# One load per group for chunk 0's queries and keys, chunk 1's groups on every second step, a third early expert

## The reference, cut to what matters

```python
# attention: 4 batches, 8 heads, 576 positions, head size 64, causal window of 64
scores = where((rel >= 0) & (rel < 64), q @ k.T / 8, -1e9)
x = softmax(scores) @ v                      # -> 2304 tokens x 512
# dense layer
h = x @ w_in                                 # 512 -> 2048
x = (h * tanh(softplus(h))) @ w_out          # 2048 -> 512
# routed layer, 8 experts of 512 -> 1024 -> 512
go  = x @ w_skip > 0                         # only these tokens are computed
e   = argmax(x @ w_gate); gate = softmax(x @ w_gate)[e]
out = x;  out[go] = x + gate * (relu(x @ w1[e]) @ w2[e])
```

## Time and profile before

| what | us |
|---|---|
| median of three runs (747.63 to 750.29) | 749.41 |
| the profiled execution | 753.54 |
| its span, first to last instruction | 752.0 |
| TensorE busy (92% of the span) | 693.8 |
| VectorE busy | 485.8 |
| ScalarE busy | 362.9 |
| GpSimd busy | 272.0 |

### The profile page before, as it was taken

One profiled execution on the slowest core, in us unless ns is written; L12 is line 12 of the kernel. 1 busy time (PEld: TensorE's weight loads), 2 busy tenths in 40 slices (PEclk: granted clock), 3 DMA queues, 4 the chain that ended last, 5 costly groups with the idle time before them and its releaser, 6 DMA issues.

```text
span 752.0 us, 13811 instructions
## 1 busy us (share of the span) xinstructions
PE 693.8 (92%) x4974; PEld 615.3 (82%) x4974; DVE 485.8 (65%) x920; ACT 362.9 (48%) x791; POOL 272.0 (36%) x238
## 2 busy tenths in 40 slices
PE   4867799999999999999999999997999889999993
PEld 3756679888888988988988988986888779999893
DVE  3453785686686686686687687678587635445360
ACT  4545445545555455455455555553454035353430
POOL 4415334344344434434335335334353232121221
PEclk9977999999999999999999999998999989999997
DMA  7624103116216415114215114101638789999940
GB/s 234 205 78 161 43 28 99 36 36 101 62 36 124 95 36 93 47 61 92 64 44 92 52 56 93 36 1 35 236 93 267 225 301 372 350 339 354 349 144 1
DMA packets 63410, 97.16 MB, mean 129 GB/s; under 512 B 23080, under 2 KB 28200, under 8 KB 63344
## 3 DMA queue, kind: packets, MB, share of 16 engines
q1 hardware_dynamic: 60176, 91.80, 41.2%
q0 software_dynamic: 3168, 4.51, 1.8%
HBM read 84.97 MB, written 13.73 MB: 131 GB/s over the span
## 4 chain that ended last, share of the span: by engine, by line
PE 73%; DVE 11%; DMA 5%; issue 4%; ACT 3%; POOL 1%; SPq 1%; POOLq 0%; DVEq 0%; ACTq 0%
PE Y L585 22%; PE H L566 14%; PE H L667 10%; PE OB L685 8%; PE PTB L566 6%; PE SB_ L531 4%; DMA tokens_of_experts<-tok_i,slot 3%; PE OB L550 2%; PE MB L613 2%; PE SB_ L539 1%; DVE n_sb L1008 1%; DVE u_sb L1019 1%; DVE u_sb L1015 1%; DVE g_sb L1024 1%; DVE u_sb L1004 1%
## 5 line engine op out<-in xcount | busy, mean ns | idle before, releaser
L1334 POOL TENSOR_TENSOR q_sb<-n_sb,r_sb 128x512 f32<-128x512 f32 x72 | 93.2, 1295 | 300.8 <-DVE u_sb L1019 223.3
L585 PE MATMUL Y<-wout_hi,g_hi 128*128 128x512 f32 x288 | 122.8, 427 | 16.1 <-ACT g_hi L803 16.0
L585 PE MATMUL Y<-wout_lo,g_hi 128*128 128x512 f32 x288 | 118.3, 411 | 0.0
L566 PE MATMUL H<-x_hi,win_hi 128*128 128x256 f32 x384 | 111.6, 291 | 0.0
L566 PE MATMUL H<-x_lo,win_hi 128*128 128x256 f32 x384 | 108.4, 282 | 0.0
L566 PE MATMUL H<-x_hi,win_lo 128*128 128x256 f32 x384 | 108.3, 282 | 0.0
L1340 POOL TENSOR_TENSOR g_lo<-g_sb,g_hi 128x512 fp32r<-128x512 f32 x72 | 95.4, 1325 | 0.8
L667 PEld LDWEIGHTS H<-xT,w 128*128 128x128 f32 x768 | 90.5, 197 | 1.9 <-issue 1.0
L667 PE MATMUL H<-xT,w 128*128 128x128 f32 x768 | 91.0, 281 | 0.8 <-ACT xT L828 0.8
L1004 DVE TENSOR_SCALAR u_sb<-e_sb 128x512 f32<-128x512 f32 x72 | 36.3, 504 | 84.3 <-ACT e_sb L788 83.8
L803 ACT CAST g_hi<-g_sb 128x512 fp32r<-128x512 f32 x72 | 44.6, 619 | 84.4 <-DVE g_sb L1024 76.4
(11 more groups left out here) (186 smaller groups left out, 1393.4 us busy)
## 6 DMA issues: line engine op xcount, KB each, us to landing
w<-moe_w SPq DMA_DIRECT2D x24, 2048.0 KB, 10.1
kT<-k_T SPq DMA_DIRECT2D x32, 256.0 KB, 3.0
vw<-v_w SPq DMA_DIRECT2D x32, 256.0 KB, 3.1
...
```

The lines of the kernel that those rows point to most:

```text
L566: last = nc.tensor.matmul(HM3[J % 3][:, f, :], wt[:, j, d, f * P:(f + 1) * P], xt[:, c % 2, d, :], start=(n == 0), stop=(n == 3 * DB - 1))
L585: last = nc.tensor.matmul(Y[t][:, :], gt[:, J % 2, lo:lo + P], wt[:, 2 * j + f, :], start=(j == 0 and f == 0 and wt is wout_hi and gt is g ...
L1334: nc.gpsimd.tensor_tensor(q_sb[:, :], n_sb[:, J % 2, :], r_sb[:, J % 2, :], ALU.mult).then_inc(q_ok, 1)
```

## The change

It has four parts.

1. **First loads.** Chunk 0's queries and keys lie side by side in one input (`qk0_T`), and come in one DMA for each group (`qk0`) in place of two; v is loaded from ScalarE's queue. SP issues 4 DMAs ahead of the first weight slices in place of 12, the slices come in another order, and GpSimd rounds four slices in place of two. The small addition in the softmax becomes a tensor_tensor with a tile `eps`.
2. **Chunk 1's groups.** Group (1, 0) is computed before the loop, the others have their scores in steps -1, 1 and 3. The first two steps get an order of their own on TensorE, ScalarE and VectorE.
3. **Three early experts.** `pick_early` is cut into `pick_first` (step 63), `pick_second` (step 64) and `pick_third` (step 71). The third is chosen after chunk 7 has been counted; its list is read and its rows gathered before the last chunk's tokens are placed. SP loads its first matrix once `pick_third` is done (`fixed`), and waits for the rows of block 3, not of block 2, before it loads block 3's weights.
4. **The end of block 1.** On TensorE the transposes of block 2's rows stand ahead of block 1's down projection. On VectorE the last split of block 1's second matrix and its two hT_lo stand inside the table's chain.

```diff
-EARLY = 2
+EARLY = 3
...
-        HI_POOL = (0, 2)
+        HI_POOL = (0, 2, 4, 1)
...
-        LO_POOL = (2, 4, 1, 5, 7, 9)
+        LO_POOL = (1, 3, 5, 7, 9)
...
         def scores_at(J):
-            if -1 <= J < NB - 1:
-                return (1, J + 1)
-            return group((J + 3) // 2 + NB) if J > 4 and J % 2 else None
+            return group((J + 3) // 2 + NB) if J >= -1 and J % 2 else None
...
             def load_first(b):
-                sp.dma_start(k0[:, b, :, :], k0_in[b, :, :, :]).then_inc(qk0_in[b], 16)
-                sp.dma_start(q0[:, b, :, :], q_in[b, :, :, :, :].rearrange("h d r w -> (h d) r w")).then_inc(qk0_in[b], 16)
-                sp.dma_start(v0[0:W, b, :], v_in[b, W:2 * W, :]).then_inc(v0_in[b], 16)
+                sp.dma_start(qk0[:, b, :, :, :], qk0_in_dram[b, :, :, :, :]).then_inc(qk0_in[b], 16)
...
             sp.wait_ge(bh_ok, 2)
-            load_w1(es[2], 0)
+            sp.wait_ge(fixed, FSTEPS)
+            third = early_expert(2)
+            load_w1(third, 0)
...
-            sp.wait_ge(xs_in[2], 16)
-            for b in range(EARLY + 1, NE):
+            sp.wait_ge(xs_in[EARLY], 16)
+            for b in range(EARLY, NE):
                 load_block(b, b // RING, b % RING)
...
# TensorE, tick(J)
-                if gs and not gp:
+                if gs and not gp and J > 1:
                     scores(*gs)
...
+                if J == 1:
+                    weigh_v(*probs_at(0))
+                    scores(*gs)
-                if gp:
+                if gp and J > 0:
                     probs_T(*gp)
                 down(J)
-                if gp:
+                if gp and J > 0:
                     weigh_v(*gp)
+                if J == 0:
+                    probs_T(*gp)
...
             for half in range(2):
                 expert_up(1, 0, 1, half)
+            rows_T(2, 0, 2)
             expert_down(1, 1, 0, EFB)
-            rows_T(2, 0, 2)
...
# VectorE
-                nc.vector.tensor_scalar(dene[:, :], den[:, :], 1e-9, None, ALU.add).then_inc(den_ok, 1)
+                nc.vector.tensor_tensor(dene[:, :], den[:, :], eps[:, :], ALU.add).then_inc(den_ok, 1)
...
                 if c == NC - 2 and j == 7:
-                    pick_early()
+                    pick_first()
+                if c == NC - 1 and j == 0:
+                    pick_second()
...
                 if c == NC - 1 and j == 7:
+                    pick_third()
                     rest_of_w2(1, 1, 0)
...
# GpSimd
+                if c == NC - 1 and j == 7:
+                    pool.wait_ge(fixed, FSTEPS)
+                    load_early(2)
...
+            pool.wait_ge(y_out[1], 128 * 5)
+            gather(0, 2)
             scatter_tokens(NC - 1)
             scatter_rows(0, 0)
-            row2 = early_list(EARLY)
             all_placed(NC - 1)
-            pool.dma_start(blk_tok[:, 2:3], tokens[bass.ds(row2, P), :]).then_inc(bt_in[2], 16)
-            pool.wait_ge(y_out[0], 128 * 6)
-            pool.wait_ge(y_out[1], 128 * 5)
-            gather(0, 2)
```

More of the change, by code:

```diff
@@ L75, in build @@
         dv = sb("dv", [P, NV])
-        early_e = sb("early_e", [P, EARLY + 1], I32)
-        early_row = sb("early_row", [P, EARLY + 1], I32)
+        early_e = sb("early_e", [P, EARLY], I32)
+        early_row = sb("early_row", [P, EARLY], I32)
+        turn = sb("turn", [P, EARLY])
+        first = sb("first", [P, EARLY, NE])
         blk_tok = sb("blk_tok", [P, RING], I32)
@@ L308, in blocks @@
         def blocks(eng, nblk, block_of):
-            for b in range(EARLY, NE):
+            for b in range(2, NE):
                 block_of(b, b // RING, b % RING)
@@ L455, in _ @@
                     sp.wait_ge(picked, PSTEPS)
-                    es = [early_expert(k) for k in range(EARLY + 1)]
+                    es = [early_expert(k) for k in range(2)]
                     sp.wait_ge(g1_ok, NJ * c + 4)
@@ L854, in tick @@
                 ahead = J + 1 < NC * NJ
-                if ahead:
+                if ahead and J > 0:
                     mish_exp(J + 1)
+                if J < 2:
+                    if J == 0:
+                        x_hi_out(1, 0)
+                    g_hi_out(J)
                 if gp:
@@ L885, in tick @@
                     expert_relu(0, 1)
+            for b in range(NB):
+                act.dma_start(v0[0:W, b, :], v_in[b, W:2 * W, :]).then_inc(v0_in[b], 16)
             nc.scalar.preload_act_table_set(EXP_AND_LOG)
@@ L1087, in pick_early @@
                 nc.vector.memset(dv[:, :], 0.0)
-                for k in range(EARLY):
-                    step(nc.vector.reduce_max(top[:, k:k + 1], held, AX.X))
-                    step(nc.vector.scalar_tensor_tensor(out=atmax, in0=held, scalar=top[:, k:k + 1], in1=rev[:, 0, :],
-                                                        op0=ALU.is_equal, op1=ALU.mult))
-                    step(nc.vector.reduce_max(turn[:, k:k + 1], atmax, AX.X))
-                    step(nc.vector.tensor_scalar(ohe[:, k, :], rev[:, 0, :], turn[:, k:k + 1], None, ALU.is_equal))
-                    if k == 0:
-                        nc.vector.tensor_scalar(taken[:, :], held, float(P), None, ALU.min)
-                        step(nc.vector.scalar_tensor_tensor(out=held, in0=ohe[:, 0, :], scalar=-float(BIG), in1=held,
-                                                            op0=ALU.mult, op1=ALU.add))
@@ L1098, in pick_early, with pick_second @@
-                step(nc.vector.tensor_scalar(enov[:, NE:NV], turn[:, :], -1.0, float(NE), ALU.mult, ALU.add))
+                nc.vector.tensor_scalar(taken[:, :], held, float(P), None, ALU.min)
+                marked(0, step)
+                strike(0, step)
+                assert count[0] == 6, count
+            def pick_second():
+                step, count = steps(picked, 6)
+                marked(1, step)
+                nc.vector.tensor_scalar(enov[:, NE:NE + 2], turn[:, 0:2], -1.0, float(NE), ALU.mult, ALU.add)
+                nc.vector.tensor_scalar(early_e[:, 0:2], turn[:, 0:2], -1.0, float(NE), ALU.mult, ALU.add)
+                nc.vector.tensor_scalar(early_row[:, 0:2], turn[:, 0:2], -float(NTOK), float(NE * NTOK), ALU.mult, ALU.add)
@@ L1113, in pick_early @@
-                assert count[0] == PSTEPS, count
+                step(nc.vector.reduce_sum(basev[:, NE:NV], first[:, :, :], AX.X))
+                assert count[0] == FSTEPS, count
             def rest_of_w2(b, slot_, k):
@@ L1148, in tick @@
                     logits_out(c - 1, 0)
-                if gp:
+                if gp and J > 0:
                     normalise(*gp)
                 mish_g(J)
+                if J == 0:
+                    soften(*scores_at(-1))
+                    normalise(*gp)
                 if route_at(c, j) == 2:
@@ L1192, in _ @@
             x_lo_out_first(2)
+            soften(1, 0)
             x_lo_out_first(3)
-            soften(1, 0)
+            rest_of_slice(2)
+            normalise(1, 0)
+            rest_of_slice(4)
+            mish_n(0)
+            rest_of_slice(6)
             dve.wait_ge(consts, 2)
-            rest_of_slice(6)
-            mish_n(0)
-            rest_of_slice(3)
+            mish_n(1)
+            x_lo_out(1, 0)
             for J in range(NC * NJ):
@@ L1246, in _ @@
             assert count[0] == TSTEPS, count
-            rest_of_w2(1, 1, 3)
-            for half in range(2):
-                rest_of_relu(1, half)
             gate_rows(1, 0, 1)
@@ L1391, in tick @@
                     nc.gpsimd.memset(blank[:, :, :], 0.0).then_inc(blank_ok, 1)
[L1392 removed]
+                if c == NC - 1 and j == 1:
                     early_tokens()
```

149 lines of the change are left out of this document (94 added, 55 removed).

## The result

The changed kernel takes 742.39 us in the median of 5 runs (740.38 to 745.00) against 749.41 (5 runs): ratio 0.9907, 95% interval 0.9882 to 0.9932. That is 7.0 us, where 16.9 were forecast.

A forecast was written before the change was run, and what follows sets the result against it. TensorE is back to back from about 110 us but waits in three stretches. Gains of 6.6 (chunk 0), 4.5 (last chunk) and 5.8 us (experts) sum to 16.9, giving a 732.5 us median; own range 728 to 737, overall 723 to 741.

The forecast's parts named there:

- block 3's weights: Turn to the experts: weights issued only after block 3's rows land, so TensorE waits 0 to 6 us, taken 2.0.
- step 4: Chunk 0, fifth pass of the loop counting from 0: keeps its order and today's 7.2 us.
- D(0): Start of down projection 0 (D(J): of loop step J): 1.1 us earlier, bounds 0.5 later to 4 earlier.
- D(0) to D(1): Chunk 0, between the first two down projections' starts: one chain of 16.2 us, 1.6 slower than before.
- D(1) to D(6): Chunk 0, steps 1 to 5 with groups every second step: 43.9 us against 50.98, 7.1 gained.
- always held: Rival: GpSimd's remainders always hold VectorE, so chunk 0 gives only 1.7 us; 737.6 us in all, chance 0.14.
- Turn to the last chunk: Split pick starts down(64) 2.9 us earlier and keeps the clock, 2.1; sum 4.5 us gained, bounds 2.5 and 5.
- Turn to the experts up to block 3: Blocks 1 and 2: waits removed 6.3 us, third pick costs 1.7, faster up 3.2; sum 7.8 us gained.
- block 3 late: Rival: three transfers share the queue, second matrix lands near 627, wait of 6 us; 736.5 us, chance 0.12.
- thirteenth block: Rival: an early expert passes a row boundary later and needs one more block, 13.2 us; 745.7 us, chance 0.03.
- the low clock: Rival: TensorE idles in D(0) to D(1), then stays at 1.2 GHz through chunk 0; 757 us, chance 0.03.
- named signs of being wrong: D(0) to D(1) under 14 us, D(6) moving under 2 or over 13 us, or later blocks waiting for weights.

The follow-up runs named there:

- e5: Changed kernel with GpSimd writing zeros in place of the remainders of slices 3, 5, 7 and 9; ratio to before 0.9859.
- e6: Changed kernel with the remainders of slices 3, 5, 7 and 9 on VectorE in place of GpSimd; ratio to before 0.9872.
- e13: Changed kernel with g_lo ahead of the next q on GpSimd in steps 0 and 1; one run, 737.29 us.
- e11: Changed kernel with e3 and e6 together; 734.34 us, ratio to before 0.9803.
- e14: e11 with e13's exchange of g_lo and q added; 728.51 us, ratio to before 0.9714.
- e1: Kernel before with only the change's loads, slice and group orders of chunk 0 and the tensor form of the addition; ratio to before 0.9978.
- e3b: Changed kernel without SyncE's wait for block 3's rows ahead of its weights; ratio to before 0.9897.
- e12: Changed kernel with the small addition ahead of each reciprocal in scalar form again; one run, 740.41 us.
- e3: Changed kernel with SyncE asking for block 3's first matrix before waiting for its rows, the second after; ratio to before 0.9827.
- e4: Changed kernel with the first loads as before, all twelve issued by SyncE; ratio to before 0.9907.
- e10: Changed kernel asking for block 3's first matrix at once and its second when GpSimd has issued the rows' gather; ratio to before 0.9919.

## Why the prediction was wrong

The places and mechanisms were mostly right, and two terms of the sum were not: block 3's weights, priced at 2.0 us and worth 9.1, and the steps of chunk 0 after D(1), with step 4 taken as one without attention. Against the forecast the profiled execution lacks 8.3 us: 3.8 in chunk 0 and 7.0 at the experts, less 0.7 at the last chunk, 1.5 in the middle and 0.3 behind.

- **D(0), 1.1 us earlier: not shown.** It varies with the execution. Seven profiles with this start have D(0) from 40.09 to 43.85, mean 42.1; two with the old one 42.85 and 41.49, mean 42.2. The first up alone (first matmul to first exponential) took 3.1 to 5.5 us by the level of TensorE's clock. The new start reaches the first up some 0.8 us sooner; the hold from slice 3's remainder, named as a possibility, came every time and cost 1.9 (e5, e6).
- **D(0) to D(1), 16.2: right**, 16.02 here and 16.26 in most variants, and by the reason given: q(1) ahead of g_lo(0) is on the chain (e13: 12.19 without it). That it was avoidable the prediction did not say.
- **D(1) to D(6), 43.9: the failing term is step 4.** The steps took 11.98, 8.70, 9.44, 9.15 and 6.48 us against 11.8, 8.6, 9.1, 7.2 and 7.2. "Steps 4 and 5 keep their order and today's 7.2 each" was wrong: with groups on every second step, the group whose scores stand in step 3 has its probabilities in step 4, which had none before. I had not followed the last group through. VectorE was held there as well (4.51 us for two remainders), but it is TensorE that sets this step: it is never idle between D(4) and D(5), and 3.4 us of it ran at the low level. The same step of e6, windows from D(4) to D(5) as above, has no low stretch and takes 7.88 us:

```profile
89.99:99.14 9.15, 9.15 (x61) 7.20 (x61) 8.91 (x11) 5.04 (x8) 4.62 (x4) 0.81 0.10 22
84.71:92.59 7.88, 7.71 (x60) 6.48 (x61) 7.32 (x10) 5.08 (x8) 3.65 (x4) 1.00 0.15 33
```

It is so in every profile with this order of groups: 7.9 us with no low stretch (e6, e11, e14; 8.3 in e5, with a wait of 0.6 for g_lo), 9.0 to 9.2 with 3.4 us of it (the changed kernel, e1, e3b, e12, e13), 10.0 to 10.1 with some 6 (e3, e4, e10). So some 0.7 of the 1.95 us missing is the group, and the rest is the clock: "TensorE at its low level is hidden, as VectorE and ScalarE set the pace" failed here. What took the clock down is not shown. TensorE had waited 2.04 us ahead of down(4) in every run where it fell, and 1.3 to 1.6 in e5, e6, e11 and e14, where GpSimd has no remainders of slices 5, 7 and 9 and the clock stayed up. Steps 1 to 3 came within 0.4 us of their forecast, holds included. Chunk 0 as a whole gave 2.8 us, near the rival "always held" (1.7 in the text; its own bounds, 0.5 + 1.6 - 4.6, make it 2.5), but what made the difference from 6.6 was D(0) and step 4.
- **Turn to the last chunk: right.** D(64) at 517.58 is 7.64 earlier, 3.1 of it since D(63) (forecast 2.9), and the clock was kept: 5.2 in all against 4.5.
- **Turn to the experts up to block 3: right in sum.** Block 2's up came 5.6 us closer to D(69) (forecast -6.3 + 1.7 = -4.6), and from there to where block 3's up was wanted 2.3 were gained (3.2): 7.9 against 7.8. The third pick cost TensorE some 1.0 us (block 0's down took 9.50 us, 8.45 before; 0.82 of it is a wait for ytile), not 1.7.
- **Block 3's weights: the mis-sized term, 9.1 us in place of 2.0, outside my 0 to 6.** Of the 9.1, 4.2 are the wait for the first matrix, 2.6 the low level of the up behind it and 2.0 the wait for hT_lo. Three errors. The low level after the wait was in no term, though the earlier trace rows had it (10.30 for 7.14). The issue came at 598.51; taken back by the 9.5 us that the program was ahead this is 608.0, not 605.4: the tokens were placed 1.6 later, and the rows took 8.3 us, not 7.3. Why the tokens were late is open in part: counted from D(69) the scatter was issued 1.1 us later than before, and the list 9.7 us behind it in place of 7.5; but e1, with the old order there, has 10.1, and the other profiles with the new order 8.2 to 10.2, so this differs between executions. (Block 2's second matrix was issued 0.3 us ahead of the scatter in both kernels.) And behind the second matrix I counted one cast and one remainder (2.3), while VectorE does four remainders ahead of hT_lo: 614.1 to 620.6 is 6.5 us. The rival "block 3 late" had the mechanism and too small a price, because I read the want of w_lo and not the order in which VectorE gets to hT_lo.

The rivals of a thirteenth block and of the low clock did not come: later block ups follow at 13.1 us as before, and chunk 0's granted clock was 0.89 from 30 to 60 us. The rivals were priced one at a time; "always held" and "block 3 late" together make 741.4 us, close to what was measured, and had no chance of their own. None of the named signs of being wrong came either (D(0) to D(1) under 14 us, D(6) moved by less than 2 or more than 13, later blocks waiting): the signs were too wide for an error of this size.
